# The column comparisons of two routing rounds, beside the FFN: four groups of three instead of nine of one or two

## The chip, the cores and the metric

The kernel runs on one core of a Trainium2 chip. The metric is the device time of one execution in microseconds (us), the median over several runs. The engines are TensorE (PE in the rows; its weight loads are PEld), VectorE (DVE), ScalarE (ACT), GpSimd (POOL) and SyncE (SP).

## The reference

Three layers, one behind the other, in float32:

```python
attn_out = _attn_ref(q, k, v, n_sink=4, window=128)     # 2 x 8 heads x 768 x 64
x = attn_out.transpose(0, 2, 1, 3).reshape(1536, 512)

# routing: 1536 tokens, 8 experts of 192 places each
logits = x @ w_gate
for idx in argsort(-logits.flatten()):                  # best pair of token and expert first
    tok, e = idx // 8, idx % 8
    if assigned[tok] >= 0 or counts[e] >= 192: continue
    assigned[tok] = e; counts[e] += 1
out[mask] = relu(x[mask] @ w1[e]) @ w2[e]               # per expert: 512 -> 1024 -> 512

h = out @ w_in                                          # the FFN: 512 -> 2048 -> 512
return (max(h, 0) + alpha * min(h, 0)) @ w_out
```

## The kernel before, in words

The routing is done in rounds: each round finds the next expert that fills up, and with it the 192 tokens of that expert. The program does the experts in the order in which they fill, two at a time. After two experts (`2j` and `2j+1`) it has 384 finished rows, and sends them through the FFN at once, so there are four FFNs, `j` = 0 to 3. In the two FFNs `j` = 0 and 1 there are two routing rounds beside the work: the rest of round `ra = 2j+2`, and then the ranking of round `rb = 2j+3`, the "second round". The ranking compares all 1536 keys with all 1536 keys, in 12 columns of 128 tokens. For a column `c`:

- VectorE's `compare(rb, c)` makes three instructions: `beats` for the elements before the column's own block (128*c of them; none for c = 0), `ties` for the block itself (128 elements), `beats` for the rest (1536 - 128*c). All read `rank_row` in SBUF and write bf16 tiles in SBUF. `beats` and `ties` are rings of three columns.
- TensorE's `count(rb, c)` waits for `beats_ready` of that column, then adds it up with 12 + 1 matmuls of 9 columns each. `compare` of column c waits until `count` of column c - 3 is done.

An FFN runs over 16 blocks `f` of 128 hidden features. TensorE does for each f, in this order: `up(f)`, 12 matmuls 128x384 (L1602), into one of two banks; `down(f - 2)`, 9 matmuls 128x512 (L1617); then `routing_beside_ffn(j, f)`, which is where `count` stands. The values are float32 taken as two parts, so the other engines have to make the parts:

- ScalarE, for each f: `g_neg` (two passes, L794 and L796) as soon as `up(f)` is done; `wi_hi` for block f + 2 (L744); `g_hi` (L801) as soon as VectorE's `g` of f is there; `wo_hi` (L749).
- VectorE, for each f: `g_lo` (L1205) and `wo_lo` (L1199) of f - 1; `g` (L1215) of f, which waits for `g_neg`; then `routing_beside_ffn(j, f)`, which is where `compare` stands.
- GpSimd, for each f up to 13: `wi_lo` for block f + 2 (L603), as soon as `wi_hi` of that block is there. The last of an FFN, for block 15, follows ScalarE's pass at f = 13.

`up(f)` waits for `g` of f - 2, and `down(f)` for `g_lo` and `wo_lo` of f. Each engine runs its list in the written order; which column is compared and counted beside which f is in two tables named `COLUMNS`, one in VectorE's list, one in TensorE's.

Of the kernel before, what the change touches and what calls it, by code (L numbers as in the profile page):

```python
# [58 lines left out]
def program(nc, q_t, k_t, k_sink, v_rows, v_sink_d, wg_d, w1_d, w2_d, w_in_d, w_out_d, alpha_d, out, n_sink, window):  # L59
# [9 lines left out]
    with ctx:  # L69
# [754 lines left out]
        def _(dve):  # L824
# [112 lines left out]
            def compare(r, c, first=0, end=3):  # L937

                def piece(lo, hi, op):
                    return nc.vector.tensor_scalar(out=beats[:, c % 3, lo:hi], in0=rank_row[:, lo:hi],  # L942
                                                   scalar1=key[:, c:c + 1], scalar2=None, op0=op)

                if c == 0 and r >= 2:
                    dve.wait_ge(row_loaded, 16 * (r - 1))
                if first == 0:
                    dve.wait_ge(counted, NT * r + c - 2)
                    if c:
                        piece(0, c * P, ALU.is_lt)  # L950
                    nc.vector.scalar_tensor_tensor(out=ties[:, c % 3, :], in0=rank_row[:, c * P:(c + 1) * P],
                                                   scalar=key[:, c:c + 1], in1=tri_after[:, :],
                                                   op0=ALU.is_equal, op1=ALU.mult)
                last = piece(max(c * P, first * 512), end * 512, ALU.is_le)
                if end == 3:
                    last.then_inc(beats_ready, 1)
# [102 lines left out]
            def token_numbers(r):  # L1059

                dve.wait_ge(picked, r + 1)
                if r >= 2:
                    dve.wait_ge(tok_moved, r // 2)
                for k, (t, rows) in enumerate(ROWS[r % 2]):
                    n, count = TURNS * (r % 2) + k, rows.stop - rows.start
                    if r >= 2:
                        dve.wait_ge(gathered[r % 2][k], 16 * (r // 2))
                    nc.vector.tensor_copy(tok_next[0:count, n:n + 1], PICKED[0:count, n:n + 1]).then_inc(tok_ready, 1)
# [33 lines left out]
            def experts(j):  # L1102
# [46 lines left out]
                for c in range(9, 11):  # L1149
# [6 lines left out]
                y_rest(r + 1, 3)  # L1156


            COLUMNS = {f: range(c, c + n) for f, c, n in ((7, 0, 1), (8, 1, 2), (9, 3, 1), (10, 4, 1), (11, 5, 2), (12, 7, 1),
                                                          (13, 8, 1), (14, 9, 2), (15, 11, 1))}  # L1160

            def routing_beside_ffn(j, f):

# [16 lines left out]
                if f == 6:  # L1180
                    token_numbers(ra)
                if f in COLUMNS and j < 2:
                    for c in COLUMNS[f]:
                        compare(rb, c)
# [43 lines left out]
        def _(pe):  # L1228
# [149 lines left out]
            def turn_keys(r):  # L1378

                pe.wait_ge(key_ready, r + 1)  # L1380
                into = M_BANK[0][0:NT, 0:P] if r in KEYS_BESIDE_FFN else KEYS
                nc.tensor.transpose(into, key[:, :], ident[:, :]).then_inc(keys_turned, 1)

            def count(r, c):
                if c == 0:
                    pe.wait_ge(want_ready, r + 1)
                    pe.wait_ge(room_ready, r)
                    pe.wait_ge(tok_ready, TURNS * r)
                    nc.tensor.matmul(COUNTS, ones[:, :], start_row[:, :, :], start=True, stop=False, skip_group_check=True)
                pe.wait_ge(beats_ready, NT * (r - 1) + c + 1)  # L1390
                for t in range(NT):
                    nc.tensor.matmul(COUNTS[:, t, :], beats[:, c % 3, t * P:(t + 1) * P], want[:, c, :],  # L1392
                                     start=False, stop=False, skip_group_check=True)
                nc.tensor.matmul(COUNTS[:, c, :], ties[:, c % 3, :], want[:, c, :], start=False,  # L1394
                                 stop=(c == NT - 1), skip_group_check=True).then_inc(counted, 1)
# [126 lines left out]
            def routing_beside_expert(r, done):  # L1522
# [21 lines left out]
                if r in (2, 4):  # L1544
# [4 lines left out]
                    if done == 8:  # L1549
                        pick_tokens(r + 1)  # L1550


            COLUMNS = {f: range(c, c + n) for f, c, n in ((8, 0, 1), (9, 1, 2), (10, 3, 1), (11, 4, 1), (12, 5, 2), (13, 7, 1),
                                                          (14, 8, 1), (15, 9, 2), (16, 11, 1))}

            def routing_after_up(j, f):

# [4 lines left out]
            def routing_beside_ffn(j, f):  # L1562
# [6 lines left out]
                if j < 2:  # L1569
                    if f == 3:  # L1570
                        turn_keys(rb)
                    if f in COLUMNS:
                        for c in COLUMNS[f]:
                            count(rb, c)
# [133 lines left out]
```

## Time and profile before

| | |
|---|---|
| median of 3 runs | 635.64 us (635.63 to 636.36) |
| profiled execution | 635.48 us, of it the span 633.6 us |
| PE busy | 614.9 us (97%) |
| DVE busy | 418.6 us (66%) |
| ACT busy | 308.5 us (49%) |
| POOL busy | 196.5 us (31%) |
| granted TensorE clock, mean | 0.996 |

The span is the time between the first and the last instruction that the profiler saw; the execution's own time has 1.88 us around it. All times below are microseconds from the span's start. TensorE's matmuls are pipelined: the next begins while the last is still draining, so their recorded durations overlap, and their pace is read from start to start.

### The profile page before, as it was taken

How to read it: one execution, taken by the hardware profiler on the slowest of the kernel's cores; microseconds unless marked ns; L12 is line 12 of the kernel's file. 1: busy time of each engine (PE TensorE's matmuls, PEld its weight loads, DVE VectorE, ACT ScalarE, POOL GpSimd, SP SyncE). 2: the span in 40 equal slices, each digit the busy share in tenths (PEclk: the TensorE clock that was granted, in tenths of full speed). 3: DMA queues.
4: the chain of work that ended last, by engine and by line, in shares of the span. 5: the costliest groups of instructions: out<-in, count | busy, mean ns of one | idle time of the engine just before them, and what ended most of it. 6: DMA issues, size and time to landing. Idle time of an engine off the chain costs nothing.

```text
span 633.6 us, 12921 instructions
## 1 busy us (share of the span) xinstructions
PE 614.9 (97%) x4942; PEld 554.5 (88%) x4947; DVE 418.6 (66%) x1156; ACT 308.5 (49%) x716; POOL 196.5 (31%) x211
## 2 busy tenths in 40 slices
PE   8799999889999999999999999999999999999996
PEld 4689998759899888899999888999988989999995
DVE  7788887988576979844759797439687520035552
ACT  5888884512132655532236554322566542346663
POOL 5998881010121342111113421201233410113331
PEclk9999999899999999999999999999999999999999
DMA  7477754535450242037003510360017610000001
GB/s 261 152 260 273 276 192 161 190 96 198 140 204 1 68 171 104 2 114 264 14 2 103 204 37 2 137 254 1 2 67 246 243 64 13 1 1 1 1 1 50
DMA packets 31220, 72.36 MB, mean 114 GB/s; under 512 B 2876, under 2 KB 2936, under 8 KB 31160
## 3 DMA queue, kind: packets, MB, share of 16 engines
q1 hardware_dynamic: 27232, 60.69, 27.2%
q0 software_dynamic: 1984, 6.29, 3.0%
q10 hardware_dynamic: 1944, 4.56, 1.9%
q8 instruction: 39, 0.64, 0.4%
q14 instruction: 21, 0.17, 0.1%
HBM read 65.22 MB, written 6.32 MB: 113 GB/s over the span
## 4 chain that ended last, share of the span: by engine, by line
PE 78%; DVE 2%; issue 0%; ACT 0%; POOLq 0%; POOL 0%; DVEq 0%
PE bank L1602 22%; PE bank L1617 21%; PE bank L1514 14%; PE bank L1505 14%; PE bank L1392 3%; PE bank L1483 1%; PE bank L1461 1%; DVE beats L971 1%; DVE beats L942 0%; PE bank L1418 0%; PE bank L1445 0%; PE bank L1233 0%; PE bank L1438 0%; PE bank L1394 0%; DVE in_slot L1055 0%
## 5 line engine op out<-in xcount | busy, mean ns | idle before, releaser
L603 POOL TENSOR_TENSOR wi_lo<-w_in,wi_hi 128x512 fp32r<-128x512 f32 x64 | 89.0, 1392 | 272.5 <-ACT wi_hi L744 272.5
L942 DVE TENSOR_SCALAR beats<-rank_row,key 128x512 bf16<-128x512 f32 (+11 forms) x144 | 92.6, 664 | 11.5 <-PE bank L1394 11.5
L1617 PE MATMUL bank<-wo_lo,g_hi 128*128 128x512 f32 x192 | 76.0, 396 | 0.0
L1617 PE MATMUL bank<-wo_hi,g_lo 128*128 128x512 f32 x192 | 75.7, 394 | 0.0
L1617 PE MATMUL bank<-wo_hi,g_hi 128*128 128x512 f32 x192 | 75.5, 393 | 0.0
L1215 DVE SCALAR_TENSOR_TENSOR g<-bank,g_neg 128x384 f32<-128x384 f32 x64 | 35.5, 555 | 52.8 <-ACT g_neg L796 52.8
L794 ACT ACTIVATE g_neg<-bank 128x384 f32<-128x384 f32 x64 | 31.4, 491 | 78.1 <-PE bank L1602 77.7
L1602 PE MATMUL bank<-y_hi,wi_hi 128*128 128x384 f32 x256 | 57.9, 347 | 0.0
L770 ACT ACTIVATE h_t<-bank 128x192 f32<-128x192 f32 x64 | 21.2, 331 | 72.8 <-PE bank L1505 72.8
L670 ACT ACTIVATE prob<-neg_s,neg_max 128x260 f32<-128x260 f32 x96 | 48.8, 509 | 15.0 <-DVE neg_max L853 12.9
L1602 PE MATMUL bank<-y_lo,wi_hi 128*128 128x384 f32 x256 | 55.2, 336 | 0.0
L1602 PE MATMUL bank<-y_hi,wi_lo 128*128 128x384 f32 x256 | 54.7, 334 | 0.0
L1205 DVE TENSOR_TENSOR g_lo<-g,g_hi 128x384 fp32r<-128x384 f32 x64 | 44.4, 694 | 14.7 <-ACT g_hi L801 14.5
L1083 DVE TENSOR_TENSOR y_lo<-bank,y_hi 128x192 fp32r<-128x192 f32 x32 | 11.3, 354 | 60.3 <-ACT y_hi L781 60.2
L781 ACT CAST y_hi<-bank 128x192 fp32r<-128x192 f32 x32 | 10.2, 319 | 77.5 <-PE bank L1514 77.5
L1514 PE MATMUL bank<-h_t,w_b 128*128 128x192 f32 x256 | 47.7, 334 | 0.0
L1602 PEld LDWEIGHTS bank<-y_hi,wi_hi 128*128 128x128 f32 x256 | 44.1, 188 | 3.4 <-ACT y_hi L781 0.2
L1602 PEld LDWEIGHTS bank<-y_lo,wi_hi 128*128 128x128 f32 x256 | 46.2, 188 | 0.0
L1505 PE MATMUL bank<-x_gt,w_b 128*128 128x192 f32 x256 | 45.3, 330 | 0.7 <-ACT x_gt L760 0.7
L1199 DVE TENSOR_TENSOR wo_lo<-w_out,wo_hi 128x512 fp32r<-128x512 f32 x64 | 45.8, 715 | 0.0
L801 ACT CAST g_hi<-g 128x384 fp32r<-128x384 f32 x64 | 32.8, 513 | 25.8 <-DVE g L1215 21.1
L1602 PEld LDWEIGHTS bank<-y_hi,wi_lo 128*128 128x128 f32 x256 | 45.4, 188 | 0.0
(180 smaller groups left out, 1359.6 us busy)
## 6 DMA issues: line engine op xcount, KB each, us to landing
w_a<-moe_w SPq DMA_DIRECT2D x8, 1024.0 KB, 5.1
w_a<-moe_w SPq DMA_DIRECT2D x4, 2048.0 KB, 10.3
w_b<-moe_w SPq DMA_DIRECT2D x8, 1024.0 KB, 5.1
w_b<-moe_w SPq DMA_DIRECT2D x4, 2048.0 KB, 10.2
k_raw<-k_t SPq DMA_DIRECT2D x11, 512.0 KB, 5.3
q_raw<-q_t SPq DMA_DIRECT2D x11, 512.0 KB, 4.0
w_in<-moe_w_in SPq DMA_DIRECT2D x8, 512.0 KB, 5.0
w_out<-moe_w_out SPq DMA_DIRECT2D x8, 512.0 KB, 4.5
```

The source lines that it names most:

```text
L603: nc.gpsimd.tensor_tensor(out=wi_lo[:, f % 2, :, :], in0=w_in[:, :, f * P:(f + 1) * P], in1=wi_hi[:, f % 2, :, :].bitcast(F32), op=ALU.sub ...
L670: nc.scalar.activation(prob[b][:, h, :], neg_s[:, h % 4, :], ACT.Exp, bias=neg_max[b][:, h:h + 1], scale=-1.0, accum_out=p_sum[b][:, h, 0: ...
L794: nc.scalar.activation(g_neg[:, :], UP_BANK[f % 2][:, 0:GS], ACT.Relu, scale=-1.0).then_inc(neg_turned, 1)
L801: nc.scalar.copy(g_hi[:, f % 3, :], g[:, f % 2, :]).then_inc(g_hi_done, 1)
L942: return nc.vector.tensor_scalar(out=beats[:, c % 3, lo:hi], in0=rank_row[:, lo:hi], scalar1=key[:, c:c + 1], scalar2=None, op0=op)
L1199: nc.vector.tensor_tensor(out=wo_lo[:, f % 2, :], in0=w_out[:, f, :], in1=wo_hi[:, f % 2, :].bitcast(F32), op=ALU.subtract).then_inc(wo_sp ...
L1205: nc.vector.tensor_tensor(out=g_lo[:, f % 3, :], in0=g[:, f % 2, :], in1=g_hi[:, f % 3, :].bitcast(F32), op=ALU.subtract).then_inc(g_split, 1)
L1215: nc.vector.scalar_tensor_tensor(out=g[:, f % 2, :], in0=u, scalar=0.0, in1=g_neg[:, :], op0=ALU.max, op1=ALU.add).then_inc(g_ready, 1)
L1505: last = nc.tensor.matmul(into, w1[e][:, c, k * P:(k + 1) * P], x_gt[e][:, c, :], start=(c == 0), stop=(c == DC - 1))
L1514: last = nc.tensor.matmul(into, w2[e][:, f, m * P:(m + 1) * P], h_t[e][:, f, :], start=(f == 0), stop=(f == EC - 1))
L1602: last = nc.tensor.matmul(UP_BANK[f % 2][:, 0:GS], w[:, f % 2, c, :], y[:, c, :], start=(n == 0), stop=(n == len(passes) - 1))
L1617: last = nc.tensor.matmul(DOWN_BANK[t][:, :], a[:, f % 3, t * P:(t + 1) * P], w[:, f % 2, :], start=(f == 0 and n == 0), stop=(f == FC - 1 ...
```

## The change

Both tables `COLUMNS` are changed and nothing else. They matter in the FFNs `j` = 0 and 1 alone.

```diff
@@ VectorE @@
-            COLUMNS = {f: range(c, c + n) for f, c, n in ((7, 0, 1), (8, 1, 2), (9, 3, 1), (10, 4, 1), (11, 5, 2), (12, 7, 1),
-                                                          (13, 8, 1), (14, 9, 2), (15, 11, 1))}
+            COLUMNS = {f: range(c, c + n) for f, c, n in ((7, 0, 2), (8, 2, 1), (10, 3, 3), (12, 6, 3), (14, 9, 3))}
@@ TensorE @@
-            COLUMNS = {f: range(c, c + n) for f, c, n in ((8, 0, 1), (9, 1, 2), (10, 3, 1), (11, 4, 1), (12, 5, 2), (13, 7, 1),
-                                                          (14, 8, 1), (15, 9, 2), (16, 11, 1))}
+            COLUMNS = {f: range(c, c + 3) for f, c in ((9, 0), (11, 3), (13, 6), (15, 9))}
```

Each entry is (f, first column, number of columns). The lines behind the tables move up by one (VectorE) or two (TensorE): L1215 becomes L1214, L1392 becomes L1391, L1602 becomes L1600.

VectorE's list in the FFN j = 0, from `g` of f = 10 on, before. It compares column 4 (512 and 1024 elements), goes on with the parts of f = 10, makes `g` of f = 11 and begins column 5:

```order
L1215 SCALAR_TENSOR_TENSOR g<-bank,g_neg 128x384
L942 TENSOR_SCALAR beats<-rank_row,key 128x512
L951 SCALAR_TENSOR_TENSOR ties<-rank_row,key,tri_after 128x128
L942 TENSOR_SCALAR beats<-rank_row,key 128x1024
L1205 TENSOR_TENSOR g_lo<-g,g_hi 128x384
L1199 TENSOR_TENSOR wo_lo<-w_out,wo_hi 128x512
L1215 SCALAR_TENSOR_TENSOR g<-bank,g_neg 128x384
L942 TENSOR_SCALAR beats<-rank_row,key 128x640
```

The same place after the change: from `g` of f = 10 to `g` of f = 11 stand the columns 3, 4 and 5.

```order
L1214 SCALAR_TENSOR_TENSOR g<-bank,g_neg 128x384
L942 TENSOR_SCALAR beats<-rank_row,key 128x384
L951 SCALAR_TENSOR_TENSOR ties<-rank_row,key,tri_after 128x128
L942 TENSOR_SCALAR beats<-rank_row,key 128x1152
L942 TENSOR_SCALAR beats<-rank_row,key 128x512
L951 SCALAR_TENSOR_TENSOR ties<-rank_row,key,tri_after 128x128
L942 TENSOR_SCALAR beats<-rank_row,key 128x1024
L942 TENSOR_SCALAR beats<-rank_row,key 128x640
L951 SCALAR_TENSOR_TENSOR ties<-rank_row,key,tri_after 128x128
L942 TENSOR_SCALAR beats<-rank_row,key 128x896
L1204 TENSOR_TENSOR g_lo<-g,g_hi 128x384
L1198 TENSOR_TENSOR wo_lo<-w_out,wo_hi 128x512
```

The parts of f = 10 and `g` of f = 11 now stand behind nine comparison instructions instead of three.

TensorE's list at the end of f = 11 in the same FFN, before: the last matmul of `down(9)`, column 4, and `up(12)`.

```order
L1617 MATMUL bank<-wo_lo,g_hi 128x512
L1392 MATMUL bank<-want,beats 128x9 x12
L1394 MATMUL bank<-want,ties 128x9
L1602 MATMUL bank<-y_hi,wi_hi 128x384 x4
L1602 MATMUL bank<-y_lo,wi_hi 128x384 x4
L1602 MATMUL bank<-y_hi,wi_lo 128x384 x4
```

The same place after the change:

```order
L1615 MATMUL bank<-wo_lo,g_hi 128x512
L1391 MATMUL bank<-want,beats 128x9 x12
L1393 MATMUL bank<-want,ties 128x9
L1391 MATMUL bank<-want,beats 128x9 x12
L1393 MATMUL bank<-want,ties 128x9
L1391 MATMUL bank<-want,beats 128x9 x12
L1393 MATMUL bank<-want,ties 128x9
L1600 MATMUL bank<-y_hi,wi_hi 128x384 x4
L1600 MATMUL bank<-y_lo,wi_hi 128x384 x4
L1600 MATMUL bank<-y_hi,wi_lo 128x384 x4
```

Columns 3, 4 and 5 stand there now; at the ends of f = 8, 10, 12, 14 and 16 no column is left.

## Rows read from the trace of the kernel before

**Rows 1.** The page: span, and busy time of TensorE and VectorE.

```profile
span 633.6 us, 12921 instructions
...
PE 614.9 (97%) x4942; PEld 554.5 (88%) x4947; DVE 418.6 (66%) x1156; ACT 308.5 (49%) x716; POOL 196.5 (31%) x211
```

**Rows 2.** Waits of TensorE: who for whom, us in total, times, longest.

```profile
PE bank L1392 <- DVE beats L942: 0.6, 1, 0.6
```

**Rows 3.** Chain that ended last, f = 8 (j = 0): start, us, what.

```profile
230.63 2.10 PE bank L1602 x12
232.73 2.09 PE bank L1617 x9
```

**Rows 4.** The same chain, f = 11 to 13.

```profile
246.93 2.09 PE bank L1617 x9
...
249.34 2.22 PE bank L1602 x12
...
253.65 0.30 PE bank L1392 x12
...
253.97 0.30 PE bank L1392 x12
...
254.29 2.19 PE bank L1602 x12
```

**Rows 5.** Timeline of all engines, f = 11 and 12: start, us, instruction.

```profile
246.97 0.49 ACT L794 ACTIVATE g_neg<-bank 128x384 f32<-128x384 f32 x1 [1.80 <-PE bank L1602]
248.02 0.61 ACT L744 CAST wi_hi<-w_in 128x512 fp32r<-128x512 f32 x1
248.62 0.55 DVE L942 TENSOR_SCALAR beats<-rank_row,key 128x640 bf16<-128x640 f32 x1
248.70 1.61 POOL L603 TENSOR_TENSOR wi_lo<-w_in,wi_hi 128x512 fp32r<-128x512 f32 x1 [3.06 <-ACT wi_hi L744]
249.08 1.39 DVE L951 SCALAR_TENSOR_TENSOR ties<-rank_row,key,tri_after 128x128 bf16<-128x128 f32 x1
250.39 1.20 DVE L942 TENSOR_SCALAR beats<-rank_row,key 128x896 bf16<-128x896 f32 x2
251.52 0.34 DVE L951 SCALAR_TENSOR_TENSOR ties<-rank_row,key,tri_after 128x128 bf16<-128x128 f32 x1
252.31 0.54 DVE L1205 TENSOR_TENSOR g_lo<-g,g_hi 128x384 fp32r<-128x384 f32 x1
252.78 0.68 DVE L1199 TENSOR_TENSOR wo_lo<-w_out,wo_hi 128x512 fp32r<-128x512 f32 x1
253.33 1.28 POOL L603 TENSOR_TENSOR wi_lo<-w_in,wi_hi 128x512 fp32r<-128x512 f32 x1 [3.01 <-ACT wi_hi L744]
253.38 0.54 DVE L1215 SCALAR_TENSOR_TENSOR g<-bank,g_neg 128x384 f32<-128x384 f32 x1
253.49 0.46 PE L1392 MATMUL bank<-want,beats 128*128 128x9 bf16 x12
253.96 0.51 ACT L801 CAST g_hi<-g 128x384 fp32r<-128x384 f32 x1 [0.70 <-DVE g L1215]
254.37 0.61 ACT L749 CAST wo_hi<-w_out 128x512 fp32r<-128x512 f32 x1
```

**Rows 6.** Timeline of VectorE and GpSimd, f = 13.

```profile
258.17 0.75 DVE L942 TENSOR_SCALAR beats<-rank_row,key 128x1024 bf16<-128x1024 f32 x1
...
258.25 1.82 POOL L603 TENSOR_TENSOR wi_lo<-w_in,wi_hi 128x512 fp32r<-128x512 f32 x1 [3.64 <-ACT wi_hi L744]
...
258.83 1.39 DVE L951 SCALAR_TENSOR_TENSOR ties<-rank_row,key,tri_after 128x128 bf16<-128x128 f32 x1
```

**Rows 7.** Timeline at the end of the first round's ranking.

```profile
127.28 0.28 DVE L971 TENSOR_SCALAR beats<-rank_row,key 128x128 bf16<-128x128 f32 x1
...
127.62 0.18 PE L1423 MATMUL bank<-want,ties 128*128 128x9 bf16 x1 [0.51 <-DVE beats L971]
```

## The prediction

> **What bounds the kernel now.** I read the page first. TensorE is busy for 614.9 of 633.6 us [rows 1]; VectorE, at 418.6 us, has room on average. Then TensorE's waits: the only one for a comparison is 0.6 us, once, outside the FFNs [rows 2]. So in the two FFNs the change touches, TensorE never stands still, and the time there is the sum of what its list holds. The chain of waits gives its pace: an `up` of 12 matmuls takes 2.10 us, a `down` of 9 takes 2.09 [rows 3], so an f without routing takes 4.19 us. With one column or two behind the `down`, a column costs 0.32 (253.65 to 253.97 to 254.29), and the `up` behind it takes 2.19 or 2.22 instead of 2.10 [rows 4]. Last I read the timeline of f = 11 to 13, to see how much room the other engines have within these 4.19 us, because the change stacks VectorE's work.
>
> I count time from the start of ScalarE's `g_neg` of an f, which comes 0.04 after the end of `up(f)` (246.97 against 246.93) [rows 4, 5]. ScalarE starts `wi_hi` at +1.05, VectorE's first comparison starts at +1.65, GpSimd's `wi_lo` at +1.73 [rows 5].
>
> VectorE and GpSimd get in each other's way there. `ties` takes 0.34 us at 251.52, and 1.39 at 249.08, right after GpSimd's `wi_lo` has begun; it ends at 250.47, just behind the `wi_lo` (248.70 + 1.61 = 250.31) [rows 5]. And `wi_lo` takes 1.28 when VectorE is in nothing of the kind (253.33), but 1.61 when it comes 0.38 before the end of a running comparison [rows 5], and 1.82 when it comes 0.58 before it (258.25 against 258.83) [rows 6]. One of the two runs, the other waits until that instruction is over. Each meeting costs VectorE 1.05 us (1.39 - 0.34). In the old order every f has at most one meeting, since VectorE is done before the next `wi_lo`.
>
> **The change, part by part.**
>
> *Fewer entries into the matmuls of 9 columns.* The columns, 12 per FFN, and their 13 matmuls each stay, at 0.32. What goes is the price per group. Before, seven groups in an FFN (f = 8 to 14) have an `up` behind them, one (f = 15) a `down`, one (f = 16) the transposes. After, three have an `up` (f = 9, 11, 13) and one the same `down`. So four `up`s get back 0.09 to 0.12, I take 0.10 [rows 3, 4]; for the exit into the transposes, of which I show no row, I take half a price, between nothing and the same 0.12. That is 0.45 per FFN, 0.9 us for two (0.7 to 1.2).
>
> *VectorE at f = 7 and 8.* Two columns, then one, instead of one, then two. They are read at the end of f = 9, 2 x 4.19 + 1.89 = 10.3 after f = 7's `g_neg`. One column costs VectorE 1.32: c5 and c6 take from 248.62 to 252.31, 3.69, less one meeting of 1.05 [rows 5]; every column covers 1536 elements and one `ties`. Three columns, two meetings and the parts between them are 1.65 + 3.96 + 2.10 + 1.07 + 0.48 = 9.3 at most. Nothing, hidden under two whole f's of TensorE.
>
> *VectorE at f = 10 and f = 12.* Three columns in a row, then the parts of f, then `g` of f + 1. Walk f = 10, t = 0 at its `g_neg`:
> - c3 begins at 1.65. GpSimd's `wi_lo` of block 12 comes at 1.73 and meets it: +1.05. c5 begins at 1.65 + 1.05 + 2 x 1.32 = 5.34. Its first `beats` (640 elements) takes 0.46 (248.62 to 249.08), its `ties` 0.26 (1.31 from 249.08 to 250.39, less 1.05) [rows 5]: they end at 5.80 and 6.06.
> - No column is counted at the end of f = 10, so f = 11's `g_neg` comes at 4.19 [rows 3], and with it `wi_lo` of block 13 at 4.19 + 1.73 = 5.92. That falls into c5's `ties`. GpSimd starts at 6.06, and the last `beats` of c5 waits for it: a second meeting, +1.05. c5 is done at 1.65 + 2 x 1.05 + 3 x 1.32 = 7.71, by its record 0.08 later (252.78 + 0.68 against the next start, 253.38) [rows 5], 7.79.
> - TensorE sees a tile of VectorE's 0.06 after its end (127.56 to 127.62) [rows 7], at 7.85.
> - TensorE after f = 10's `up`, which ends at -0.04: down 2.09, up 2.10, down 2.09, end at 6.24; records of the first count start 0.16 earlier (253.49 against 253.65) [rows 4, 5], at 6.08. c3 and c4 are there, and take 0.65. At 6.73 it wants c5 and stands until 7.85: **1.1 us**.
>
> f = 12 goes the same way with c6 to c8. c8 begins at 5.34, its first `beats` (1024 elements) takes 0.66 (258.17 to 258.83) [rows 6], to 6.00; `wi_lo` of block 15 comes at 5.92 into it, and its `ties` waits. End again 7.71, wait again 1.1. That the second walk starts clean: the late c5 moves f = 12's `g_neg` to about 7.85 + 0.16 + 0.33 + 2.19 + 0.04 = 10.57. VectorE has `g` of f = 11 at 7.71 + 1.07 = 8.78 (`g_lo` 0.47, `wo_lo` 0.60), ScalarE follows with `g_hi` at 9.36 and `wo_hi` until 10.38 [rows 5]. So ScalarE is free 0.19 before it is wanted. `down(10)` wants `wo_lo` at 10.5 and has it at 8.86.
>
> f = 14 holds c9 to c11, and no `wi_lo` is left by then (the last comes at f = 13). 1.65 + 3.96 = 5.61, against 6.08 at the earliest. Nothing.
>
> So two waits of 1.1 in each of two FFNs, 4.4 us (between nothing, if GpSimd does not come between, and 2 x 1.05 each if a third meeting crept in). TensorE is the bound and has nothing else to do there, so the whole wait is in the span.
>
> **The pages on this.** What decides is who gets the pair first when GpSimd asks in the middle of VectorE's run of nine instructions. In the rows GpSimd has it at the next boundary: its 1.82 and 1.61 us are 1.28 and the rest of one instruction, with two more comparisons already in VectorE's list [rows 5, 6]. The Trainium skill, page SBUF — State Buffer, section Who interferes with whom, says that the pair of ports shared by the two is an exclusive lock: whichever instruction issues first holds it to its end and the other fully blocks. If queued comparisons counted as issued, that rule would let GpSimd wait out the whole run, c5 would be there before TensorE asks, and the sum would be the gain of 0.9 us alone, 634.6; the rows say one instruction, so I go by them.
>
> **Sum.** +4.4 - 0.9 = +3.5 us on the profiled execution's 635.48: 639.0. The median of the runs shown is 0.16 higher (635.64), within what I can tell. About 0.2%, 1.3 us, is what a measurement of this kernel tells from no change.
>
> **The rivals.**
> - *Only one meeting per group.* f = 10's margin is thin: `wi_lo` has to come before 6.06 and comes at 5.92 by my sum. If it comes later, the last `beats` runs first, and c5 is there at 1.65 + 1.05 + 3.96 + 0.08 + 0.06 = 6.80, practically on time. f = 12 has 0.34 of margin (up to the end of c8's `ties`, 6.26). f = 12 alone colliding gives 2.2 - 0.9 = +1.3: 636.8. Chance 0.12.
> - *No second meeting at all*, because VectorE's pace keeps the pair, or because my clock is off by a third of a microsecond. Then only the exits count, and a wait under 0.1 four times: about -0.7, 634.8, not slower. It decides at one point: whether the `wi_lo` of the next f runs inside the third column. Against it speak the two `wi_lo` that started after one instruction [rows 5, 6]. Chance 0.13.
>   The lock rule of the Trainium skill, read so that a queued run holds the pair, would be this rival.
> - *Faster by more than 0.2%.* It needs no second meeting, and exits worth 0.13 or more each. The largest exit shown is 0.12. Chance 0.03.
> - *It builds up.* The 0.19 of ScalarE's room at f = 12 is used up, `g` of f = 12 comes late, and c8 with it; each group at f = 12 waits up to 0.5 longer: 640.0. Chance 0.05.
> - Two meetings in each group as above: 0.67, with 638.2 to 639.8 as its own range.
>
> **How the numbers follow.** The likeliest gives 639.0. Leaving out the cases without a second meeting (0.16) puts the low end at 636.6; the high end, 640.3, takes in the build-up. Slower by over 0.2% are the first case, the build-up and half of the 0.12: 0.78. Within 0.2%: the other half and nearly all of the 0.13: 0.18. Faster: 0.04.
>
> **What would show it.** TensorE's waits should have four for `beats` of about 1.1 us, all at a third column, at f = 11 and 13 of both FFNs, and none at f = 9 and 15. GpSimd's `wi_lo` of blocks 13 and 15 should start within VectorE's third column, and one comparison there should take 1.05 longer: the 896-element `beats` of c5, `ties` of c8. The `up`s of f = 9, 11, 13 and 15 (their `down` has no column behind it at f - 1) should take 2.10. If the four waits are absent, my clock of GpSimd's second call was wrong; if they are there and smaller, the price of a meeting or TensorE's arrival was.

## The result, and the profile after

The changed kernel takes 640.37 us (median of 4 runs, 638.74 to 640.90) against 635.63 (4 runs): ratio 1.0072, 95% interval 1.0048 to 1.0095. It is slower, by 0.7%. Measured again beside 29 runs of the kernel before, it took 639.88 against 636.25, ratio 1.0061 (1.0047 to 1.0074), which is 3.9 us (3.0 to 4.7). The profiled execution took 638.74, 3.26 more than the one before.

The page of the changed kernel, span and busy times:

```profile
span 637.0 us, 12926 instructions
...
PE 615.9 (97%) x4947; PEld 556.5 (87%) x4947; DVE 418.5 (66%) x1156; ACT 308.6 (48%) x716; POOL 194.7 (31%) x211
```

Against [rows 1], the span is 3.4 us longer, VectorE is as busy as before and TensorE only 1.0 us busier, and that in a stretch ahead of every changed line (112 to 144 us: 28.80 us busy against 27.64, shown below). So TensorE stood still for longer. Its waits (total, times, longest) for the comparisons of the rounds beside the work:

```profile
PE bank L1391 <- DVE beats L942: 4.3, 5, 0.9
```

In [rows 2] this was 0.6, once. The list of TensorE's waits also has three for comparisons of the first round, 1.5 us in total (the one of [rows 7] is among them), in both kernels alike and ahead of the FFNs; the prediction left them out when it called the 0.6 the only one. The four new ones are 3.7 us, 0.9 each. To place them I take the chain that ended last, for the FFN j = 0, from `up(7)` to the first matmuls of the next filler (`x2`, the end of the stage):

```profile
226.15 2.30 PE bank L1600 x12
...
234.72 2.10 PE bank L1600 x12
...
242.16 0.50 ACT g_neg L794
...
250.44 2.23 PE bank L1600 x12
...
252.69 0.50 ACT g_neg L794
...
265.29 2.10 PE bank L1600 x12
...
275.73 0.22 PE bank L1437 x2
```

The same two ends in the chain of the kernel before:

```profile
226.24 2.30 PE bank L1602 x12
...
274.10 0.22 PE bank L1438 x2
```

The stage takes 49.58 us after, 47.86 before: 1.72 longer. The FFN j = 1 takes 49.57 by the same ends, against 47.86. The stage begins at the same time in both (226.15 against 226.24), so nothing ahead of it was lost. The two stages, 1.72 and 1.71, are the 3.4 of the span. The `up`s of f = 9 and f = 15, which have no column ahead of them now, take 2.10.

Inside f = 10 and 12 the timeline of VectorE, GpSimd and TensorE shows, with what each waited for in brackets:

```profile
243.81 0.41 DVE L942 TENSOR_SCALAR beats<-rank_row,key 128x384 bf16<-128x384 f32 x1
243.89 1.48 POOL L603 TENSOR_TENSOR wi_lo<-w_in,wi_hi 128x512 fp32r<-128x512 f32 x1 [4.02 <-ACT wi_hi L744]
244.14 1.38 DVE L951 SCALAR_TENSOR_TENSOR ties<-rank_row,key,tri_after 128x128 bf16<-128x128 f32 x1
...
247.95 0.34 DVE L951 SCALAR_TENSOR_TENSOR ties<-rank_row,key,tri_after 128x128 bf16<-128x128 f32 x1
248.08 1.34 POOL L603 TENSOR_TENSOR wi_lo<-w_in,wi_hi 128x512 fp32r<-128x512 f32 x1 [2.71 <-ACT wi_hi L744]
248.21 1.69 DVE L942 TENSOR_SCALAR beats<-rank_row,key 128x896 bf16<-128x896 f32 x1
249.82 0.55 DVE L1204 TENSOR_TENSOR g_lo<-g,g_hi 128x384 fp32r<-128x384 f32 x1
249.96 0.46 PE L1391 MATMUL bank<-want,beats 128*128 128x9 bf16 x12 [0.91 <-DVE beats L942]
...
258.61 1.29 POOL L603 TENSOR_TENSOR wi_lo<-w_in,wi_hi 128x512 fp32r<-128x512 f32 x1 [2.50 <-ACT wi_hi L744]
258.70 1.35 DVE L951 SCALAR_TENSOR_TENSOR ties<-rank_row,key,tri_after 128x128 bf16<-128x128 f32 x1
...
260.50 0.46 PE L1391 MATMUL bank<-want,beats 128*128 128x9 bf16 x12 [0.91 <-DVE beats L942]
```

Here is the walk of the prediction as it ran. GpSimd's second `wi_lo` comes 5.92 after f = 10's `g_neg` (248.08 - 242.16), inside c5's `ties`, and c5's last comparison takes 1.69 instead of about 0.67. c5 is done at 7.66, TensorE begins it at 7.80 (249.96 - 242.16). At f = 12 the same `wi_lo` again comes at 5.92 (258.61 - 252.69), and it is c8's `ties` that takes 1.35.

### The profile page after: what moved, and what is told of

It is laid out like the page before. It is cut to its first block, busy times and chain, and to the rows that moved or that the text cites. A ratio compares the mean times of both kernels' runs of the same rounds, so it can differ in the third digit from the quotient of the medians.

```text
span 637.0 us, 12926 instructions
## 1 busy us (share of the span) xinstructions
PE 615.9 (97%) x4947; PEld 556.5 (87%) x4947; DVE 418.5 (66%) x1156; ACT 308.6 (48%) x716; POOL 194.7 (31%) x211
## 4 chain that ended last, share of the span: by engine, by line
PE 73%; DVE 6%; ACT 1%; issue 1%; POOLq 0%; POOL 0%
PE bank L1600 20%; PE bank L1615 18%; PE bank L1513 14%; PE bank L1504 13%; PE bank L1391 3%; DVE beats L942 3%; DVE beats L971 1%; DVE ties L951 1%; PE bank L1482 1%; PE bank L1460 1%; PE bank L1232 1%; PE bank L1444 0%; ACT g_neg L796 0%; DVE g L1214 0%; PE bank L1437 0%
## 5 line engine op out<-in xcount | busy, mean ns | idle before, releaser
L603 POOL TENSOR_TENSOR wi_lo<-w_in,wi_hi 128x512 fp32r<-128x512 f32 x64 | 87.1, 1363 | 273.9 <-ACT wi_hi L744 273.9
L1214 DVE SCALAR_TENSOR_TENSOR g<-bank,g_neg 128x384 f32<-128x384 f32 x64 | 35.4, 553 | 53.2 <-ACT g_neg L796 53.2
L1600 PE MATMUL bank<-y_hi,wi_hi 128*128 128x384 f32 x256 | 57.2, 345 | 0.0
L1600 PE MATMUL bank<-y_lo,wi_hi 128*128 128x384 f32 x256 | 55.2, 337 | 0.0
L1600 PE MATMUL bank<-y_hi,wi_lo 128*128 128x384 f32 x256 | 54.8, 334 | 0.0
L1600 PEld LDWEIGHTS bank<-y_hi,wi_hi 128*128 128x128 f32 x256 | 44.7, 188 | 4.1 <-ACT y_hi L781 0.2
L1600 PEld LDWEIGHTS bank<-y_lo,wi_hi 128*128 128x128 f32 x256 | 46.3, 188 | 0.0
L1600 PEld LDWEIGHTS bank<-y_hi,wi_lo 128*128 128x128 f32 x256 | 45.4, 188 | 0.0
```

What stands on the lines that cost most here:

```text
L603: nc.gpsimd.tensor_tensor(out=wi_lo[:, f % 2, :, :], in0=w_in[:, :, f * P:(f + 1) * P], in1=wi_hi[:, f % 2, :, :].bitcast(F32), op=ALU.sub ...
L1214: nc.vector.scalar_tensor_tensor(out=g[:, f % 2, :], in0=u, scalar=0.0, in1=g_neg[:, :], op0=ALU.max, op1=ALU.add).then_inc(g_ready, 1)
L1600: last = nc.tensor.matmul(UP_BANK[f % 2][:, 0:GS], w[:, f % 2, c, :], y[:, c, :], start=(n == 0), stop=(n == len(passes) - 1))
```

## The experiments

A useful measure beside the medians is the length of one FFN stage, between the two ends above, since it leaves out what varies from run to run elsewhere. For the kernel before it is 47.86 us, for the changed one 49.58.

**The changed kernel again.** No edit.

> The changed kernel once more, to settle the size: its profile shows +3.4 us of span, its other three runs were 1 to 2 us above that. Theory (four waits of 1.07 us, less 0.9 us of exits): 3.4 to 3.6 us above the kernel before. Rival (something outside the two FFNs is slower too, by what the other three runs show): 4.7 us or more above it. If the extra comes from the granted clock between 112 and 144 us, before any changed line, it should come and go in both kernels.

Measured: 639.88 against 636.25 us, ratio 1.0061 (1.0047 to 1.0074); the same four waits of 0.9. The difference of the medians is 3.6, within the first theory's 3.4 to 3.6, and the interval, 3.0 to 4.7, just takes in the 4.7 of the rival. Single runs spread by 2.8 us in the kernel before and 1.7 in the changed one. The granted clock does go down in both kernels between 112 and 144 us, ahead of every changed line; these are the windows of that stretch, in the kernel before and in the changed one (length, busy us and instructions of each engine, then the clock, DMA share, GB/s):

```profile
112.00:144.00 32.00, 27.64 (x370) 20.64 (x374) 28.48 (x109) 11.49 (x21) 2.19 (x3) 0.95 0.45 148
```

```profile
112.00:144.00 32.00, 28.80 (x367) 20.94 (x366) 27.95 (x108) 11.46 (x21) 2.19 (x3) 0.89 0.44 139
```

So the mean clock of a run mixes in this stretch. What put three of the first four runs 1.3 to 2.2 us above the profiled one can't be placed, since they left no trace. Their mean granted clock was lower, 0.987 to 0.990 against 0.992, but that alone doesn't order the times: in the second measurement a run at 0.989 took 638.89 and one at 0.995 took 639.85.

**GpSimd kept out of the third column.**

```diff
                 for f in range(FC):
+                    if j < 2 and f in (11, 13):
+                        pool.wait_ge(wo_split, FC * j + f)
                     if f + 2 < FC:
                         split_wi(j, f + 2)
```

> As the changed kernel, but GpSimd waits with wi_lo of blocks 13 and 15 until VectorE has made wo_lo of f = 10 and f = 12, so that it cannot come into the third column. Theory (the waits are the second meeting with GpSimd): TensorE's waits at f = 11 and 13 fall from 0.9 to under 0.1 each, and the time is 0.7 to 0.9 us below the kernel before. Rival (nine comparison instructions in a row are too long in themselves, whatever GpSimd does): the waits stay near 0.9 each and the time stays 3.4 us or more above it.

Measured: 635.68 against 636.25 us, ratio 0.9990 (0.9980 to 1.0000), which is 0.6 us below the kernel before (0 to 1.3). TensorE's waits are back to those of [rows 2]:

```profile
PE bank L1393 <- DVE beats L944: 0.6, 1, 0.6
```

And in its timeline the last comparison of c5 runs in its own time, with GpSimd behind `wo_lo`:

```profile
249.81 0.67 DVE L944 TENSOR_SCALAR beats<-rank_row,key 128x896 bf16<-128x896 f32 x1
...
251.63 1.29 POOL L603 TENSOR_TENSOR wi_lo<-w_in,wi_hi 128x512 fp32r<-128x512 f32 x1 [4.67 <-DVE wo_lo L1200]
```

The stage takes 47.51 us (227.75 to 275.26), 2.07 less than in the changed kernel. Nine comparisons in a row cost next to nothing, 0.09 us of the stage (47.51 against the 47.42 of the next experiment, which has no nine in a row); the second meeting with GpSimd was the loss. `wi_lo` of block 13 comes at 7.86 instead of 5.92, and nobody waits for it.

**One column an f earlier on VectorE.** TensorE's table stays that of the change.

```diff
-            COLUMNS = {f: range(c, c + n) for f, c, n in ((7, 0, 2), (8, 2, 1), (10, 3, 3), (12, 6, 3), (14, 9, 3))}
+            COLUMNS = {f: range(c, c + n) for f, c, n in ((7, 0, 2), (8, 2, 1), (9, 3, 1), (10, 4, 2), (11, 6, 1), (12, 7, 2),
+                                                          (13, 9, 1), (14, 10, 2))}
```

> TensorE's four groups of three stay, at f = 9, 11, 13, 15; VectorE compares one column an f earlier: c3 at f = 9, c4 and c5 at f = 10, c6 at 11, c7 and c8 at 12, c9 at 13, c10 and c11 at 14. Theory: c5 and c8 are done 5.3 us after g_neg of their f, TensorE wants them at 6.7, so it waits for nothing, and what is left is the gain of fewer groups, 0.9 us below the kernel before. The single column waits for count of three columns earlier, at the end of its f, which delays it by 0.8 us and nothing behind it. Rival (grouping on TensorE costs something by itself, such as a slower up behind three columns): not below the kernel before.

Measured: 635.68 against 636.25 us, ratio 0.9995 (0.9985 to 1.0005). No wait for a comparison in the FFNs. The chain, same two ends:

```profile
226.89 2.30 PE bank L1600 x12
...
274.31 0.22 PE bank L1437 x2
```

47.42 us, 0.44 less than the kernel before. That is the price of the five exits that the grouping saves in an FFN, measured with nothing else moved against it; the prediction had 0.45. Over both FFNs 0.9 us is 0.14% of the run, and the medians can't tell it from nothing.

**VectorE in threes, TensorE reading each third column one f later (e4).**

```diff
-            COLUMNS = {f: range(c, c + 3) for f, c in ((9, 0), (11, 3), (13, 6), (15, 9))}
+            COLUMNS = {f: range(c, c + n) for f, c, n in ((9, 0, 2), (10, 2, 1), (11, 3, 2), (12, 5, 1), (13, 6, 2), (14, 8, 1),
+                                                          (15, 9, 2), (16, 11, 1))}
```

> VectorE's groups of three stay as in the changed kernel, TensorE reads each third column one f later: groups of two and one, eight in an FFN (f = 9 to 16). Theory: the second meeting still happens and c5 and c8 are still done 7.7 us after g_neg, but they are wanted at 10.4, so no wait; with two up exits fewer than the kernel before the time is 0.1 to 0.3 us below it. Rival (VectorE's late g, g_lo and wo_lo hold up TensorE too): waits for g_lo or wo_lo or g appear at down(10), up(13), down(12), and the time is over 1 us above the kernel before.

Measured: 635.90 against 636.25 us, ratio 1.0001 (0.9991 to 1.0011); the stage takes 47.80 (228.41 to 276.21), no waits. The stage is 0.06 us shorter than in the kernel before, 0.12 for two, at the lower edge of what was expected and too little for the medians to show. The reason was not the expected one: the second meeting did not take place. f = 10 now has column 2 behind it, so f = 11's `g_neg` is 0.4 later, and GpSimd's request comes into c5's last comparison instead of its `ties`:

```profile
250.19 0.67 DVE L942 TENSOR_SCALAR beats<-rank_row,key 128x896 bf16<-128x896 f32 x1
250.45 2.64 POOL L603 TENSOR_TENSOR wi_lo<-w_in,wi_hi 128x512 fp32r<-128x512 f32 x1 [3.11 <-ACT wi_hi L744]
250.79 0.54 DVE L1204 TENSOR_TENSOR g_lo<-g,g_hi 128x384 fp32r<-128x384 f32 x1
251.26 0.67 DVE L1198 TENSOR_TENSOR wo_lo<-w_out,wo_hi 128x512 fp32r<-128x512 f32 x1
```

So this run doesn't separate the two theories on VectorE's late parts. It showed how near the meeting was to not happening, and led to the next.

**Useless work that makes the changed kernel faster (e5).** The changed kernel, and one matmul of zeros on TensorE at f = 10. `keep_clock(n, bank)` makes n such matmuls, 128x512 in bf16.

```diff
+                    if f == 10:
+                        keep_clock(1, M_BANK[1])
                     if f in COLUMNS:
                         for c in COLUMNS[f]:
                             count(rb, c)
```

> The changed kernel with one useless matmul of zeros (128x512, bf16) behind down(8) at f = 10, in both FFNs. It makes f = 11's g_neg, and with it GpSimd's wi_lo of block 13, 0.2 to 0.3 us later: 6.1 to 6.25 after f = 10's g_neg, that is behind the end of c5's ties (6.06). Theory (the wait at f = 11 hangs on this meeting alone): c5 is done at about 6.8, TensorE wants it at 7.0, the wait of 0.9 at f = 11 is gone, the one at f = 13 stays; an FFN gets 0.75 us shorter although TensorE has more to do, 1.5 us less than the changed kernel in all, 2.0 above the kernel before. Rival (the wait is VectorE's load, or GpSimd's instruction takes the pair wherever it comes): the wait stays or moves, and an FFN gets 0.3 us longer. Whether GpSimd then starts behind c5's last comparison or, as behind the one column of the third experiment's neighbour, only behind g_lo and wo_lo, is open.

Measured: 638.50 against 635.91 us, ratio 1.0033 (1.0018 to 1.0048), 2.1 us above the kernel before, where the changed one was 3.9. TensorE's waits for comparisons:

```profile
PE bank L1391 <- DVE beats L942: 2.4, 3, 0.9
```

Two of the four are gone, those at f = 11. The timeline around c5:

```profile
248.44 0.34 DVE L951 SCALAR_TENSOR_TENSOR ties<-rank_row,key,tri_after 128x128 bf16<-128x128 f32 x1
248.70 0.67 DVE L942 TENSOR_SCALAR beats<-rank_row,key 128x896 bf16<-128x896 f32 x1
248.78 2.83 POOL L603 TENSOR_TENSOR wi_lo<-w_in,wi_hi 128x512 fp32r<-128x512 f32 x1 [2.92 <-ACT wi_hi L744]
249.30 0.54 DVE L1204 TENSOR_TENSOR g_lo<-g,g_hi 128x384 fp32r<-128x384 f32 x1
```

GpSimd's request comes 0.08 after c5's last comparison has begun, and now it is GpSimd that waits. The stage takes 48.69 us (226.63 to 275.32), 0.89 less than the changed kernel's, with one matmul more in it.

**The same at f = 12, one matmul or two.** As the last, and:

```diff
+                    if f == 12:
+                        keep_clock(1 + j, M_BANK[1])
```

> As e5, and at f = 12 one useless matmul more in the first FFN, two in the second. Each makes GpSimd's wi_lo of block 15 about 0.22 later. First FFN: it comes at 6.15 to 6.2 after f = 12's g_neg, inside c8's ties (6.00 to 6.26). Second FFN: at 6.35 to 6.45, inside c8's last comparison (6.26 to 6.65). Theory: in the first GpSimd still goes ahead of the last comparison, and TensorE's wait at f = 13 only shrinks by what the matmul filled, from 0.9 to 0.7; in the second the last comparison is running already, the wait is gone, and GpSimd gets the pair only behind wo_lo, with a wi_lo of 2.5 us or so, as in e4 and e5. Rival (the meeting is a matter of load, not of the instant): both waits shrink alike, by 0.2 and 0.4.

There is one execution of each, 638.22 and 635.84 us, so the times are not compared; the two FFNs are, within the one trace. Both came out as the theory had them. This is the timeline at c8, first in the FFN j = 0 (one matmul), then in j = 1 (two):

```profile
259.84 1.33 POOL L603 TENSOR_TENSOR wi_lo<-w_in,wi_hi 128x512 fp32r<-128x512 f32 x1 [2.72 <-ACT wi_hi L744]
259.96 1.49 DVE L942 TENSOR_SCALAR beats<-rank_row,key 128x512 bf16<-128x512 f32 x1
261.51 0.46 PE L1391 MATMUL bank<-want,beats 128*128 128x9 bf16 x12 [0.69 <-DVE beats L942]
...
384.68 0.47 DVE L942 TENSOR_SCALAR beats<-rank_row,key 128x512 bf16<-128x512 f32 x1
384.77 2.61 POOL L603 TENSOR_TENSOR wi_lo<-w_in,wi_hi 128x512 fp32r<-128x512 f32 x1 [2.94 <-ACT wi_hi L744]
```

With one, GpSimd asks 0.12 ahead of the last comparison, which takes 1.49, and the wait is 0.69. With two, it asks 0.09 behind its start, the comparison takes 0.47, and there is no wait. 0.21 us of difference in the request decides over the whole of it. A load on VectorE would have shown in both.

**GpSimd's instruction in two halves.** The changed kernel, with `wi_lo` made as two instructions of 128x256 in the FFNs j = 0 and 1. By the edit these are blocks 9 to 15, two more than the expectation names; blocks 12 to 15 are those of the two groups.

```diff
+                if j < 2 and f >= 9:
+                    nc.gpsimd.tensor_tensor(out=wi_lo[:, f % 2, 0:2, :], in0=w_in[:, 0:2, f * P:(f + 1) * P],
+                                            in1=wi_hi[:, f % 2, 0:2, :].bitcast(F32), op=ALU.subtract)
...
```

> The changed kernel, with wi_lo of blocks 11 to 15 of the two FFNs made in two instructions of half the size, 0.65 us each if their time goes by elements. Theory (a meeting costs what is left of GpSimd's instruction): VectorE gets the pair back after the first half, and a meeting of 1.05 us becomes one of about 0.4, or two of 0.4 where the second half comes again into the same column; c5 and c8 are done 0.5 to 1.2 us earlier, and TensorE's four waits of 0.9 fall to between 0 and 0.5. Rival (the pair goes from one GpSimd instruction straight to the next): the waits stay at 0.9 or grow by the second instruction's start.

Measured: 639.57 against 635.91 us, ratio 1.0060 (1.0036 to 1.0084), which can't be told from the 1.0061 of the changed kernel. The traced execution is one of two at 642.9 us; the other four took 638.14 to 639.70. A meeting with one half does cost less, 0.49 (0.83 against 0.34), but there are two of them for each `wi_lo`, as the timeline shows; the second half of the `wi_lo` of f = 11 fell on `g_lo`:

```profile
246.25 0.83 DVE L958 SCALAR_TENSOR_TENSOR ties<-rank_row,key,tri_after 128x128 bf16<-128x128 f32 x1
...
251.33 1.08 DVE L1211 TENSOR_TENSOR g_lo<-g,g_hi 128x384 fp32r<-128x384 f32 x1
...
262.10 0.46 PE L1398 MATMUL bank<-want,beats 128*128 128x9 bf16 x12 [1.02 <-DVE beats L949]
```

So c5 was done at 7.06 instead of 7.66 and the wait at f = 11 fell to 0.31, and then it came back. TensorE was 0.6 sooner with `up(12)`, but VectorE was not sooner with `g` of f = 11, which comes behind the blocked `g_lo` (at 8.66, against 8.73 in the changed kernel). ScalarE does `g_hi` and `wo_hi` behind that `g`, and only then `g_neg` of f = 12, which is what the chain shows:

```profile
253.51 0.51 ACT g_hi L808
254.03 0.52 ACT wo_hi L756
254.55 0.40 ACT g_neg L801
```

By TensorE's own pace that `g_neg` could have begun at about 9.9 (c5 counted from 7.2, then 0.16 + 0.33 + 2.2); it began at 10.28. So f = 12 started some 0.35 late on VectorE, both halves of the next `wi_lo` fell into c8, and TensorE waited 1.02. The late start is at most 0.35 of that. The two halves, 0.49 each, fell into c8 because its `ties` and its last comparison were both still ahead, where c5 had only the last comparison left. The late start is the build-up that the prediction had as a rival.

## Why the prediction was right

*Each column and its matmuls stay, the exits go.* 0.45 per FFN was forecast. One column an f earlier, which keeps TensorE's groups and has no waits, gives 0.44.

*Nothing at f = 7 and 8, nothing at f = 14.* No wait at f = 9 or 15 in the changed kernel.

*The second meeting at f = 10.* Forecast: GpSimd at 5.92, c5 done at 7.71, seen by TensorE at 7.85. In the trace 5.92, 7.66 and 7.80. The place was certain in the walk by 0.14 us, and the matmul of zeros showed that this margin is real: 0.2 us later, and the wait is gone.

*The second meeting at f = 12.* The same figures, and a margin of 0.34, which one matmul did not use up and two did.

*The size of a wait.* 1.1 was forecast, and that TensorE's waits would list 1.1. They list 0.91. The list counts the engine's idle time, from the end of the last record; the time lost is from the moment when c5 would have begun, 6.73, to 7.80, which is 1.07. Two of these less 0.44 are 1.70, and the stage became 1.72 longer. Only the reading of the list was off.

*f = 12 starts clean.* ScalarE was forecast free 0.19 before `g_neg` of f = 12. In the changed kernel it is idle for 0.19 before it, as its row shows, and f = 12 repeats f = 10 to 0.02 (c8 done at 7.68).

```profile
252.69 0.49 ACT L794 ACTIVATE g_neg<-bank 128x384 f32<-128x384 f32 x1 [0.19 <-PE bank L1600]
```

The build-up did not happen in the change, and happened when GpSimd's instruction was cut in two.

*The sum.* +3.5 was forecast. The stages give 3.43, the spans 3.4, the profiled executions 3.3, the measurement with the most runs 3.9 (3.0 to 4.7). The median of the first four runs, 640.37, is 0.07 above the upper end of what was given, 640.3; by the ratio, 1.0072 times the 635.64 of before, it is 640.2 and just inside. The upper end was put there for the build-up, and neither trace of the changed kernel has one: c8 is done within 0.02 of c5's time, and all four waits are 0.91. So the mechanism explains 3.4 of the 4.7 us between the first medians. The rest is the part that could not be placed, and that the range took it in was luck.

*Who gets the pair.* The prediction took from the rows that GpSimd has it at VectorE's next boundary, and this held where it was used: at c3, c5, c6 and c8 of the changed kernel, in both FFNs. It doesn't hold in general, see below. The rule of the Trainium skill (SBUF — State Buffer, Who interferes with whom) is that whichever instruction issues first holds the pair to its end and the other fully blocks. The second meetings agree with it by their start times: where GpSimd asked 0.08 or 0.09 us behind the comparison's start it waited, and where it asked 0.09 to 0.13 ahead of it VectorE did. The reading under which a queued run would count as issued is excluded by the meetings at c3 and c6, where GpSimd asked 0.08 behind the start of the first of nine comparisons and had the pair before the second. Who is next when one engine already waits does not come out of the rule: after the matmul of zeros GpSimd asked at 248.78, `g_lo` started at 249.30, and `g_lo` ran first.

## What to carry to other kernels

When work is stacked on an engine that has room on average, walk one period of it with the start times of the other engines' instructions, and not only with durations: here three columns of 1.32 us fitted into two periods of 4.19, and what didn't was another engine's next instruction, which came 0.14 us too early. A loss that hangs on an instant can be taken away by moving the instant: a wait on the engine that nobody waits for took it all back. Grouping work on the bound engine saved 0.44 us per FFN as forecast, so a price per switch, counted in the chain of waits, was a good guide here to what there was to win.

## What the runs showed of the hardware that I had not expected

- GpSimd's request does not always win the next boundary. Where it came into a comparison with `ties` or another comparison next, it had the pair at its end (0.38 and 0.58 us of waiting in [rows 5, 6]). In e4, in e5 and with one or two matmuls it came into the last comparison of a column, with `g_lo` and `wo_lo` next, and VectorE ran both before it, nine times of nine: `wi_lo` took 2.64 when it asked 0.34 before the end, and 2.83 and 2.61 with the matmuls of zeros. That is each time VectorE's whole rest up to `wo_lo` and the 1.28 of the instruction, to 0.05. But what stands next on VectorE does not decide it alone. In the run with two halves the second half asked 0.44 before the end of c5's last comparison (250.89 against 251.33), again with `g_lo` and `wo_lo` next, and had the pair ahead of `g_lo`, which took 1.08; the same in the second FFN. What makes the difference was not found.
- TensorE's clock after a wait. In the run with two halves, granted clock by stretch (last but two of each row), around the wait of 1.02:

```profile
255.00:260.00 5.00, 5.00 (x26) 4.46 (x25) 4.65 (x9) 3.72 (x7) 1.88 (x2) 1.00 0.02 7
260.00:262.50 2.50, 1.48 (x42) 1.13 (x40) 2.50 (x5) 0.03 (x1) 1.66 (x2) 1.00 0.00 0
262.50:265.90 3.40, 3.40 (x17) 3.38 (x14) 2.30 (x5) 1.03 (x2) 0.00 (x0) 0.63 0.00 0
```

  TensorE was busy for 1.48 of 2.5 us, and then had 0.63 of its clock for 3.4 us, a mix of the levels 2.4 and 1.2 GHz; the `up` there took 3.30 instead of 2.21. The same came in the second FFN (3.56). With the `down` behind it (2.54 instead of 2.08) the dip cost 1.55 us, and as much in the second FFN. The two executions of this kernel at 642.9 us have a mean clock of 0.982, the other four 0.987 to 0.993. In the two profiles of the changed kernel the waits of 0.91 had no such dip behind them. If some of its other executions had one, that would account for their extra time; it is not shown.
- The exit price was paid behind 9-column matmuls and not behind a wide one. An `up` behind 13 of them took 2.19 to 2.23; behind a 128x512 matmul of zeros in bf16 it took 2.08, and the matmul itself 0.23. Both kinds are bf16; what in the narrow ones costs the 0.1 us was not looked for.
